# Event order of an interleaved attention and MLP stage, with part of the weight splitting moved to VectorE

## The reference

```python
keep = is_sink | in_window
scores = np.where(keep, scale * (q @ k.T), -1e9)
a = softmax(scores); x = a @ v                  # then (B*S, H*D) = (1536, 512)
h = np.maximum(x @ w_in, 0.0)                   # layer 1
x = h * h @ w_out
h = x @ w_in2                                   # layer 2
P = a[0] + a[1]*h + a[2]*h**2 + a[3]*h**3
Q = 1.0 + abs(b[0])*abs(h) + abs(b[1])*h**2
return (P / (Q + 1e-6)) @ w_out2
```

## Time and profile before

| | us |
|---|---|
| median of 3 runs (654.59, 656.54 and 702.28) | 656.54 |
| the profiled execution, its own time | 654.59 |
| its span, first to last instruction | 652.8 |
| busy TensorE matmul, weight load | 640.9, 599.4 |
| busy VectorE, ScalarE, GpSimd | 448.5, 392.3, 280.4 |
| mean granted TensorE clock, of full speed | 0.999 |

### The profile page before, as it was taken

How to read it: one execution, slowest core, us unless ns; L and a number is a source line. 1 busy time by engine, 2 the same in 40 slices (tenths; PEclk the granted TensorE clock), 3 DMA queues, 4 the chain that set the end, 5 groups by cost and what they waited for, 6 DMA issues and landing times.

```text
span 652.8 us, 10456 instructions
## 1 busy us (share of the span) xinstructions
PE 640.9 (98%) x3798; PEld 599.4 (92%) x3798; DVE 448.5 (69%) x694; ACT 392.3 (60%) x867; POOL 280.4 (43%) x314
## 2 busy tenths in 40 slices
PE   8989999999999999999999989999999999999997
PEld 6869999999999999999999989888999999999995
DVE  5644555455655545443577689999898989898995
ACT  4655665456555554443322277678777787778774
POOL 3998451000000000000122258777777777777773
PEclk9999999999999999999999999999999999999999
DMA  7864511051111221000234310011100210001001
GB/s 246 279 191 167 168 41 41 1 181 63 40 41 42 97 81 49 10 1 1 97 121 120 118 60 2 2 29 69 50 0 1 97 49 2 1 0 50 1 1 53
DMA packets 28971, 43.49 MB, mean 67 GB/s; under 512 B 4080, under 2 KB 19440, under 8 KB 28400
## 3 DMA queue, kind: packets, MB, share of 16 engines
q1 hardware_dynamic: 28912, 42.74, 19.8%
HBM read 36.44 MB, written 6.29 MB: 65 GB/s over the span
## 4 chain that ended last, share of the span: by engine, by line
PE 86%; DVE 10%; POOL 2%; issue 1%; ACT 1%; DVEq 0%; ACTq 0%; POOLq 0%
PE h_ps L1309 25%; PE y_ps L1321 21%; PE y_ps L1599 15%; PE s_ps L1309 7%; PE o_ps L1309 4%; DVE s_ps L992 3%; PE o_ps L1419 3%; PE s_ps L1363 2%; PE s_ps L1376 2%; DVE o_ps L992 2%; DVE p_buf L995 2%; DVE p_buf L986 1%; PE s_ps L1359 1%; DVE h_ps L992 1%; PE h_ps L1298 1%; PE o_ps L1428 1%
## 5 line engine op out<-in xcount | busy, mean ns | idle before, releaser
L1309 PE MATMUL h_ps<-xT,weights 128*128 128x384 f32 x960 | 189.3, 339 | 0.3 <-DVE sq L1002 0.3
L1309 PEld LDWEIGHTS h_ps<-xT,weights 128*128 128x128 f32 x960 | 167.4, 188 | 4.1 <-issue 2.7
L1321 PE MATMUL y_ps<-hid,weights 128*128 128x384 f32 x768 | 154.4, 341 | 0.0
L1599 PE MATMUL y_ps<-weights,hid 128*128 128x512 f32 x576 | 144.4, 395 | 2.3 <-POOL hid L607 1.0
L514 POOL TENSOR_SCALAR weights<-weights_raw 128x1024 fp32r<-128x1024 f32 x24 | 25.3, 1053 | 264.9 <-DMA weights_raw<-in_w_pack 264.7
L1321 PEld LDWEIGHTS y_ps<-hid,weights 128*128 128x128 f32 x768 | 133.8, 188 | 0.9 <-issue 0.9
L1599 PEld LDWEIGHTS y_ps<-weights,hid 128*128 128x128 f32 x576 | 107.2, 188 | 24.3 <-POOL hid L607 2.3
L690 ACT ACTIVATE sq<-sq 128x384 f32<-128x384 f32 x64 | 33.6, 525 | 116.4 <-DVE sq L1002 116.4
L607 POOL TENSOR_TENSOR hid<-p_buf,hid 128x384 fp32r<-128x384 f32 x63 | 64.7, 1028 | 40.0 <-ACT hid L875 39.7
L992 DVE RECIPROCAL s_ps<-q_buf 128x384 f32<-128x384 f32 x31 | 79.4, 2561 | 3.2
L598 POOL TENSOR_TENSOR q_buf<-h_abs,q_buf 128x384 f32<-128x384 f32 x64 | 65.0, 1016 | 34.4 <-ACT q_buf L663 31.9
(11 more groups left out here) (120 smaller groups left out, 842.6 us busy)
## 6 DMA issues: line engine op xcount, KB each, us to landing
weights_raw<-in_w_pack SPq DMA_DIRECT2D x32, 512.0 KB, 4.2
bk_raw<-in_k_pack SPq DMA_DIRECT2D x24, 256.0 KB, 3.5
q_pair<-in_q_pack SPq DMA_DIRECT2D x21, 256.0 KB, 3.5
bv<-in_v_pack SPq DMA_DIRECT2D x24, 128.0 KB, 2.1
y_scratch<-xT SPq DMA_DIRECT2D x2, 1536.0 KB, 6.2
xT<-y_scratch SPq DMA_DIRECT2D x2, 1536.0 KB, 6.4
out_y<-out_stage SPq DMA_DIRECT2D x3, 768.0 KB, 3.5
inv_cols<-in_q_pack SPq DMA_DIRECT2D x3, 256.0 KB, 3.7
```

The source lines that it names most:

```text
L1309: ins = nc.tensor.matmul(bank, weights[:, i, wp, W_IN, t * P:(t + 1) * P], x, start=(t == 0 and n == 0), stop=(t == KC - 1 and n == 2))
L1321: ins = nc.tensor.matmul(y_ps[:, m, 0:NT], weights[:, i, wp, W_OUT, m * P:(m + 1) * P], hid[:, i % 2, gp, :], start=(i == 0 and n == 0), s ...
L1599: ins = nc.tensor.matmul(y_bank(turn, t), hid2[:, i % RING, gp, t * P:(t + 1) * P], weights[:, i, wp, W_OUT, :], start=(i == 0 and n == 0) ...
```

## The change

1. **Event order.** The lists are made anew. Pair 15's A event moves behind `first1(0, 0)`, into block 0, and its B event into half 1 of iteration 0. B 17, B 20 and A 23 sit one half later than before. X qt stands in the half after M qt and ahead of the B event there; L qt follows in that half, where it was one or two halves later.
2. **Which part of an iteration does what.** ScalarE now does every X in `step`, before the exp and the copy of that half's B event; before, X of the first two tiles of a block came in `later`. VectorE does `sums` and every L in `later`, after `hidden(i + 1)`; before, `sums` and the L of a block's last tile came in `step`. M stays in `later` on VectorE.
3. **Weights.** The low parts of weight tiles 8 to 15 are taken from GpSimd and done by VectorE, one at the end of each of iterations 1 to 8 of block 0 (`weight_low_late`), as soon as ScalarE's copy of the same iteration is done and GpSimd has finished tiles 0 to 7.

```diff
--- before.py
+++ after.py
@@ -219,34 +219,37 @@
         def done_at(s):
             return [qt for qt in range(QT) if slots_before(qt) == s]
 
-        def steps(blk):
-
-
-
-            first = PAIRS * QT * (blk + 1) + 1 if blk else LEAD // 2
-            found = [("B", first)]
-            for p in range(first + 1, PAIRS * QT * (blk + 2) + 2):
+        def steps():
+
+
+            found = []
+            for p in range(LEAD // 2, P_ALL + 2):
+                qt = p // PAIRS - 1
                 found.append(("A", p))
-                if p < PAIRS * QT * (blk + 2) + 1:
+                if p % PAIRS == 1:
+                    found += [("M", qt), ("X", qt)]
+                    if qt % QT == QT - 1:
+                        found.append(("L", qt))
+                if p <= P_ALL:
                     found.append(("B", p))
+                if p % PAIRS == 1 and qt % QT < QT - 1:
+                    found.append(("L", qt))
                 if p % PAIRS == 0:
-                    found.append(("F", p // PAIRS - 1))
+                    found.append(("F", qt))
             return found
 
         def halves_of(blk):
 
-
-
-            halves = [[] for _ in range(2 * FT)]
-            for e, (kind, n) in enumerate(steps(blk)):
-                half = e + (e // 14 if blk else min(e, 1) + e // 6)
+            found = steps()
+            ends = [found.index(("L", QT * (b + 2) - 1)) + 1 for b in range(BLOCKS - 1)]
+            halves, e, gap = [[] for _ in range(2 * FT)], -1, 14 if blk else 6
+            for kind, n in found[ends[blk - 1] if blk else 0:ends[blk]]:
+                if kind in "ABF" or (kind == "L" and n % QT == QT - 1):
+                    e += 1
+                half = e + e // gap
+                if kind == "X":
+                    half = e + 1 + (e + 1) // gap
                 halves[half].append((kind, n))
-                if kind == "A" and n % PAIRS == 1:
-                    qt = n // PAIRS - 1
-                    at_once = half + 2 - half % 2
-                    halves[half].append(("M", qt))
-                    halves[at_once if qt % QT == QT - 1 else half + 1].append(("X", qt))
-                    halves[at_once if qt % QT == QT - 1 else half + 3].append(("L", qt))
             return halves
 
         def events(blk, i, half):
@@ -514,9 +517,9 @@
                 pool.tensor_scalar(weights[:, i, HI, :, :], weights_raw[i][:, LO, :], 1.0, 0.0,
                                    ALU.mult, ALU.add).then_inc(w_high, 1)
 
-            def weight_low(i, high, count):
-
-                pool.wait_ge(high, count)
+            def weight_low(i):
+
+                pool.wait_ge(w_high, i + 1)
                 for n in range(4):
                     c, cols = n // 2, slice(n % 2 * DM // 2, (n % 2 + 1) * DM // 2)
                     raw = weights_raw[i][:, LO, c * DM + n % 2 * DM // 2:c * DM + (n % 2 + 1) * DM // 2]
@@ -566,19 +569,16 @@
             def banded():
                 for i in range(6):
                     weight_high(0, i)
-                    weight_low(i, w_high, i + 1)
+                    weight_low(i)
                 pool.wait_ge(ks_loaded, 16)
                 split_earlier(EARLY)
                 weight_high(0, 6)
-                weight_low(6, w_high, 7)
+                weight_low(6)
                 split_kq(EARLY)
                 split_earlier(EARLY + 1)
                 weight_high(0, 7)
-                weight_low(7, w_high, 8)
+                weight_low(7)
                 split_kq(EARLY + 1)
-                for i in range(EARLY_W, FT):
-                    weight_low(i, w_high_late, i - EARLY_W + 1)
-
             def full():
                 for loaded in (*k_loaded[0:2], *q_loaded[0:2], bv_loaded[0]):
                     pool.wait_ge(loaded, 16)
@@ -774,12 +774,10 @@
                             spread(n // PAIRS - 1)
                     if kind == "F":
                         inv_copy(n)
-                    if kind == "X" and n % QT == QT - 1:
+                    if kind == "X":
                         x_high(n)
 
                 def later(kind, n):
-                    if kind == "X" and n % QT < QT - 1:
-                        x_high(n)
 
                     if kind == "B" and n % 2 and EARLY + 2 <= n // 2 + 2 < GROUPS:
                         split_high(n // 2 + 2)
@@ -793,7 +791,6 @@
                     slot(s)
                     for qt in done_at(s):
                         tile_out(qt)
-                step("A", LEAD // 2)
                 square(0, 0)
                 hidden(0, 0)
 
@@ -1001,6 +998,14 @@
                     dve.wait_ge(mm1_done, blk * FT + i + 1 + CREDIT)
                     nc.vector.tensor_scalar(sq[:, i % 2, :], h_ps[:, 0:NT], 0.0, None, ALU.max).then_inc(h_read, 1)
 
+                def weight_low_late(i):
+                    dve.wait_ge(w_high_late, i - EARLY_W + 1)
+                    dve.wait_ge(w_ready, EARLY_W)
+                    nc.vector.tensor_tensor(weights[:, i, LO, :, :].rearrange("p c n -> p (c n)"),
+                                            weights_raw[i][:, LO, :],
+                                            weights[:, i, HI, :, :].rearrange("p c n -> p (c n)").bitcast(F32),
+                                            ALU.subtract).then_inc(w_ready, 1)
+
                 def bias(kind, first, last, of):
                     return nc.vector.tensor_scalar(band_bias[:, kind, first:last], of, MASKED / SCALE,
                                                    -MASKED / SCALE, ALU.mult, ALU.add)
@@ -1111,16 +1116,15 @@
                     if kind == "A" and n < P_ALL:
                         scores(2 * n)
                         scores(2 * n + 1)
-                    if kind == "A" and n % PAIRS == 0:
-                        sums(n // PAIRS - 1)
                     if kind == "B":
                         pT_part(2 * n - 2)
-                    if kind == "L" and n % QT == QT - 1:
-                        x_low(n)
 
                 def later(kind, n):
-                    if kind == "A" and n % 2 == 0 and EARLY + 2 <= n // 2 + 1 < GROUPS:
-                        split_low(n // 2 + 1)
+                    if kind == "A":
+                        if n % PAIRS == 0:
+                            sums(n // PAIRS - 1)
+                        if n % 2 == 0 and EARLY + 2 <= n // 2 + 1 < GROUPS:
+                            split_low(n // 2 + 1)
                     if kind == "M":
                         divide(n)
                     if kind == "B" and n == PAIRS * KT + 6:
@@ -1128,7 +1132,7 @@
                         nc.vector.tensor_tensor(bkT[D:P, :, 0:SINK_CAP], bk_raw[D:P, :, 0:SINK_CAP],
                                                 bkT[D:P, :, 0:SINK_CAP].bitcast(F32), ALU.subtract
                                                 ).then_inc(ks_ready, 1)
-                    if kind == "L" and n % QT < QT - 1:
+                    if kind == "L":
                         x_low(n)
 
                 links[0] = common_links
@@ -1161,6 +1164,8 @@
                         if more:
                             for kind, n in events(blk, i, 0) + events(blk, i, 1):
                                 later(kind, n)
+                            if blk == 0 and 0 < i <= FT - EARLY_W:
+                                weight_low_late(i + EARLY_W - 1)
                         elif i >= 2:
                             weight_low(1, i - 2, w_ready)
                     if not more:
```

## The result

| | us |
|---|---|
| changed kernel, median of 4 runs (666.07 to 667.27) | 666.62 |
| kernel before, on the same chip, median of 4 runs | 656.63 |
| ratio, undisturbed runs alone, 95% interval | 1.0163 (1.0137 to 1.019) |
| span of the profiled execution | 664.8 (was 652.8) |

The change makes the kernel 1.6% slower. The forecast was 666.0. (One run of before, 702.28 us, fell in a slower state of the chip and is left out of the ratio.) The medians differ by 10.0 us and the two profiled executions (666.64 and 654.59) by 12.0, because the other runs of before took 656.5 us and more.

The account below looks back on a forecast made before the run. TensorE, busy 640.9 of 652.8 us, was taken as the bound. Terms -1.9 + 5.2 + 3.2 + 4.3 = +10.8 us gave 665.4 on the profiled 654.59 and 667.3 on the median 656.54; forecast 666.0, range 657 to 671.5.

Parts of the forecast that it names:

- Start, -1.9: Start of layer 1: `first1(0, 0)` no longer stands behind pair 15, so `first1(0, 2)` comes 1.9 us earlier.
- X ahead of B, +5.2: X 4, 6, 7, 9, 10: X waits for `divide` ahead of B's copy on ScalarE, delaying TensorE; 5 x 1.05 us.
- L of the last tile, +3.2: Block ends: L behind `hidden(15)` on VectorE delays the first `first1` of blocks 1 to 3; 3 x 1.1 us.
- Weights on VectorE, +4.3: Block 0: subtractions wait for ScalarE's weight copy, with scores and `relu` queued behind on VectorE; 4.3 us, bounds 0 to 10.4.
- sums, counted at 0, at most 1.5: `sums` in `later` puts `spread` back by up to 0.5 us at F 3, F 8, F 11; 0, at most 3 x 0.5.
- rival 2: Weight move costs nothing, as VectorE without GpSimd's contention catches up: 661.1 us; chance 0.17 with its neighbours (656 to 661.5).
- Rival 1: Iterations 1 to 9 of block 0: VectorE sets the pace, over 2% slower, 673.0 us; chance 0.17.

Follow-up runs that it names:

- start_alone: Kernel before with one edit: pair 15's A event behind `first1(0, 0)` and its B event in half 1 of iteration 0; 653.23 us, ratio 0.9970.
- x_after_b: Changed kernel with X of a block's first two tiles back behind B's exp and copy on ScalarE; 662.07 us.
- m_in_step: Changed kernel with `divide` (M) done by VectorE in `step`, right after its A event's scores, X still ahead of B; 661.42 us.
- l_in_step: Changed kernel with L of a block's last tile back in `step` on VectorE, ahead of `relu(15)`; 663.15 us.
- weights_lag: Changed kernel with VectorE's weight subtractions one iteration later, at the end of iterations 2 to 9; 662.74 us.
- weights_alone: Kernel before with only the low parts of weight tiles 8 to 15 moved to VectorE, at the end of iterations 1 to 8; 659.81 us, ratio 1.0069.
- weights_on_gpsimd: Changed kernel with the low parts of weight tiles 8 to 15 back on GpSimd; 662.91 us.

## Why the prediction was right

The forecast was 666.0 with +10.8 us as its sum, made on the profiled execution's 654.59; measured were 666.62 and 12.0 us more span. The mechanism held at every place that it named. The sum was 1.2 us too small, and 666.0 came nearer than that because it was set between two bases (665.4 and 667.3), which is luck. The runs also tell more than the 2% that the prediction granted them: the interval of the ratio is 0.5% wide. Term by term:

- **Start, -1.9.** Measured -2.0 in the traces, and by start_alone, which is 0.3% faster than before.
- **X ahead of B, +5.2.** By starts it is 1.03 us at A 22 and 1.11 to 1.18 at the four places in blocks 1 and 2, 5.6 in all, where the prediction took 1.05 for each; x_after_b takes back 5.4, m_in_step 6.0. The step that put the price on the wait for `divide` and not on X's own time is shown by the latter.
- **L of the last tile, +3.2.** Measured 3.3 by l_in_step; by starts 1.09 us at each block's first `first1` and about 0.1 more at its second, which goes with L too.
- **Weights on VectorE, +4.3.** Measured 4.3 by weights_lag. The laid-out places were B 18 (+1.3 forecast, 1.22 measured by starts, 72.07 against 70.85), `first1(0, 8)` and F 4 (+1.4 together, +1.47 measured, -0.36 to +1.11), B 22 (+1.6, and with A 22's 1.03 in the same stretch 2.62 measured, so 1.6).
- **sums, counted at 0, at most 1.5.** Measured 0.6: F 3 lost 0.44 us in this trace (0.34 to 0.82 in the others with this order), since `hidden(2)` and the addition behind it ran beside GpSimd and took 0.72 and 0.59 us. The addition (0.17 us in rows without GpSimd) was the part that I hadn't seen coming. F 8 and F 11 lost nothing.
- **Not in the sum at all:** 0.4 us in layer 2, below.

The Trainium skill's rule on an instruction with two inputs beside GpSimd ("SBUF — State Buffer", "Who interferes with whom") was right on its own ground: over the window of 50 to 110 us `hidden` has a mean of 577 ns in the changed kernel and 796 ns before. But where the subtraction stood in VectorE's queue decided: rival 2 named this rule, and weights_alone is 0.7% slower.

Rival 1, VectorE as the engine that sets the pace, lost: three of eight iterations had a long wait, as laid out, and each long wait gave the next iteration its slack back. How near it was to the other outcome isn't tested; no kernel with slower subtractions was run.

## What to carry to other kernels

- When one engine is almost never idle (here 97 to 98% busy), moving an instruction is free or costly by one question: what is queued behind it, on the engine that does it, while it waits? Write down the end of its input, the time to the end of the next thing that the busy engine needs from that queue, and compare with the start in the trace. Here that gave each of the waits that the prediction laid out within 0.2 us.
- Work that depends on another engine's last job of an iteration belongs one iteration later. The lag cost no buffer and gave back all 4.3 us.
- A wait inside a queue can be mended at either end: put it behind what others need, or make its input earlier. For X ahead of B both took 5 to 6 us away.

## What the hardware showed

- **A small one-input addition on VectorE is stretched by GpSimd too.** `sums` adds a constant to 128x8 numbers, from SBUF to SBUF. It takes 0.17 us with GpSimd idle and 0.73 us beside GpSimd's subtraction in weights_on_gpsimd (85.32, above). The Trainium skill, "SBUF — State Buffer", section "Who interferes with whom", says that `tensor_scalar` can run in a mode that uses both ports and then contends with GpSimd. The stretch in the trace fits that; which mode ran isn't shown by it.
- **Layer 2 differs by 0.4 us with nothing changed in it.** The loss begins with one instruction of VectorE, the fourth 128x384 reciprocal of layer 2. Before, it starts 0.10 us after the end of the instruction ahead of it:

```profile
392.65 0.61 DVE L986 SCALAR_TENSOR_TENSOR p_buf<-p_buf,consts,s_ps 128x384 f32<-128x384 f32 x1
...
393.36 2.56 DVE L992 RECIPROCAL s_ps<-q_buf 128x384 f32<-128x384 f32 x1
```

In the changed kernel VectorE stands idle for 0.46 us there, though the last input from ScalarE was written at 403.99:

```profile
403.46 0.53 ACT L671 ACTIVATE q_buf<-q_buf 128x384 f32<-128x384 f32 x1 [0.19 <-POOL q_buf L598]
...
404.45 0.62 DVE L983 SCALAR_TENSOR_TENSOR p_buf<-p_buf,consts,s_ps 128x384 f32<-128x384 f32 x1
...
405.52 2.56 DVE L989 RECIPROCAL s_ps<-q_buf 128x384 f32<-128x384 f32 x1 [0.46 <-DVE p_buf L983]
```

Some 15 us later TensorE is 0.35 to 0.37 us behind. The same reciprocal stands idle for 0.46 us in all eight kernels that have the weight subtractions on VectorE (702 VectorE instructions; it is the 515th in each), and in none of the four that have them on GpSimd (694), where it is 0.10 us as at the other reciprocals. The subtractions themselves are some 300 us earlier. Why this one instruction is late isn't shown.
- **The start varies.** The first MLP input was ready at 40.1 to 41.4 us in twelve traces, which is why differences are told here from `first1(0, 2)` on.
